# Transposes of the identity on TensorE between the second weight units and ahead of two later waits

## The reference

```python
# layer 1: attention of x [8, 8, 512, 64] with a state of 32 rows per head -> 4352 tokens of 512 values
# layer 2: soft mixture, 8 experts with 4 slots each (32 slots)
logits = x @ phi                        # [4352, 32]
d = softmax over the tokens (logits)
slot_input = (d.T @ x).reshape(8, 4, 512)
for e in range(8):
    h = np.maximum(slot_input[e] @ w1[e], 0.0)     # w1[e] 512 x 1024
    slot_out[e] = h @ w2[e]                        # w2[e] 1024 x 512
c = softmax over the slots (logits)
x = c @ slot_out
# layer 3: each token goes to the one expert that x @ w_gate names
out[mask] = gate_w * sigmoid(x @ w_output_gate)[e] * (np.maximum(x[mask] @ v1[e], 0.0) @ v2[e])
```

## Time and profile before

| | |
|---|---|
| median of three runs | 513.64 us |
| the profiled execution, whole | 512.83 us |
| its span, first to last instruction | 511.1 us |
| PE busy in the span | 452.8 us (89%) |
| mean clock granted to TensorE | 0.957 of full speed |
| data moved | 88.35 MB, mean 173 GB/s |

### The profile page before, as it was taken

How to read it: one execution, slowest core, us unless ns; L and a number is a source line. 1 busy time by engine, 2 the same in 40 slices (tenths; PEclk the granted TensorE clock), 3 DMA queues, 4 the chain that set the end, 5 groups by cost and what they waited for, 6 DMA issues and landing times.

```text
span 511.1 us, 10146 instructions
## 1 busy us (share of the span) xinstructions
PE 452.8 (89%) x3556; PEld 252.6 (49%) x3557; DVE 136.3 (27%) x278; ACT 143.9 (28%) x330; POOL 139.6 (27%) x207
## 2 busy tenths in 40 slices
PE   3788886799877949699999999999999999999991
PEld 3466664563415526544554545455454545545440
DVE  1489899830000894210101101010110101101000
ACT  3687764300000454321221212122121212212110
POOL 3153423046000122402323233232323323232110
PEclk9899999889797887999999999999999999999997
DMA  9879536748999979778674010110101011010110
GB/s 254 290 255 381 191 128 224 312 167 330 430 431 426 395 270 392 270 252 271 212 241 159 27 48 24 48 44 27 46 26 47 28 43 43 27 48 21 43 43 2
DMA packets 29378, 88.35 MB, mean 173 GB/s; under 512 B 6142, under 2 KB 15362, under 8 KB 26272
## 3 DMA queue, kind: packets, MB, share of 16 engines
q1 hardware_dynamic: 24304, 77.27, 40.8%
q0 software_dynamic: 3952, 10.33, 5.9%
q10 hardware_dynamic: 1088, 0.26, 0.3%
HBM read 77.61 MB, written 10.59 MB: 173 GB/s over the span
## 4 chain that ended last, share of the span: by engine, by line
PE 76%; DMA 8%; DVE 7%; issue 4%; ACT 2%; POOL 1%; SPq 0%; POOLq 0%; DVEq 0%; ACTq 0%
PE bank L874 48%; DMA arena<-in_moe_w 7%; PE bank L863 3%; PE bank L862 3%; PE bank L777 3%; PE bank L729 3%; PE bank L529 2%; PE bank L540 2%; PE bank L521 1%; DVE rsum L1120 1%; PE bank L557 1%; DVE rmx L1089 1%; DVE z L1093 1%; DVE nbias L1110 1%; PE bank L765 1%
## 5 line engine op out<-in xcount | busy, mean ns | idle before, releaser
L874 PE MATMUL bank<-arena,z 128*128 x560 | 249.2, 598 | 1.4 <-DVE z L1384 0.8
L874 PEld LDWEIGHTS bank<-arena,z 128*128 128x128 f32 x560 | 103.6, 190 | 122.5 <-issue 120.5
L1384 DVE TENSOR_SCALAR z<-bank 128x512 f32<-128x512 f32 x35 | 24.2, 691 | 251.3 <-PE bank L863 251.3
L1051 ACT ACTIVATE z<-bank,tile_gate 128x512 f32<-128x512 f32 x35 | 24.0, 687 | 228.3 <-PE bank L874 228.3
L460 POOL COPY rows_to<-sidx 128x1 int32 (+1 forms) x35 | 6.3, 181 | 152.9 <-ACT z L1051 152.9
L468 POOL DMA_INDIRECT z<-token_rows,rows_from x36 | 37.9, 1054 | 29.0 <-POOL rows_from L460 29.0
L478 POOL DMA_INDIRECT out<-z,rows_to x35 | 35.7, 1019 | 29.8 <-POOL rows_to L460 29.8
L862 PE MATMUL bank<-cT,parts 128*128 128x128 bf16 x280 | 36.4, 219 | 0.5 <-issue 0.5
L863 PE MATMUL bank<-cT,parts 128*128 128x128 bf16 x280 | 36.5, 219 | 0.0
L862 PEld LDWEIGHTS bank<-cT,parts 128*128 x280 | 27.4, 98 | 1.2 <-issue 0.9
L863 PEld LDWEIGHTS bank<-cT,parts 128*128 x280 | 27.4, 98 | 1.0 <-issue 0.5
(11 more groups left out here) (226 smaller groups left out, 498.4 us busy)
## 6 DMA issues: line engine op xcount, KB each, us to landing
arena<-in_moe_w SPq DMA_DIRECT2D x31, 2048.0 KB, 11.3
arena<-in_x SPq DMA_DIRECT2D x8, 1024.0 KB, 6.3
parts<-in_moe_w SPq DMA_DIRECT2D x1, 2048.0 KB, 8.6
token_rows<-z SPq DMA_DIRECT2D x8, 162.0 KB, 2.2
z<-token_rows,rows_from POOLq DMA_INDIRECT x36, 2.6
out<-z,rows_to POOLq DMA_INDIRECT x35, 2.9
z<-in_state ACTq DMA_DIRECT2D x4, 64.0 KB, 3.0
z<-in_state SPq DMA_DIRECT2D x4, 64.0 KB, 2.7
```

Of the source, the lines that this page charges most:

```text
L874: mm = e.matmul(pY[p][:, :], hT[p][:, c, :], arena[:, bass.ds(ex * UNIT + 512 * c, 512)], start=(c == 0), stop=(c == CF - 1))
L1051: e.activation(ysb[p], pY[p][:, :], ACT.Copy, scale=tile_gate[:, q:q + 1])\
L1384: e.tensor_scalar(hT[p][:, 4:8, :], bank[2 * p + 1][:, :].rearrange("p (c t) -> p c t", c=4), 0.0, None, ALU.max).then_inc(relu_v, 1)
```

## The change

Seven blocks of 14 transposes are put between the eight second units, 4 transposes behind the last of them (ahead of the wait for `so_copied`), and 4 ahead of the wait for `sot_ready`. Together 106 transposes are added. Nothing is removed and no wait is added.

```diff
                 mm.then_inc(w_used, 1)
+                if ex < NE - 1:
+                    keep_clock(14, pL)
+            keep_clock(4, pL)
             e.wait_ge(so_copied, 1)
             for c in range(CD):
                 mm = e.matmul(pT[:, P * c:P * c + P], every(soP, c, CD), fold[:, :, :], start=True, stop=True)
             mm.then_inc(sot_psum, 1)
 
+            keep_clock(4, pE)
             e.wait_ge(sot_ready, 1)
```

## The result

The changed kernel takes 518.31 us in the median of 11 runs (515.88 to 520.45), the kernel before 513.7 us in 11 runs beside it (512.11 to 515.71). The ratio is 1.0081, with a 95% interval of 1.0057 to 1.0106: the change costs 4.2 us (2.9 to 5.4). The forecast was 518.5.

What follows compares the result with a forecast made beforehand. The bound was the wait chain from second units through gate matmuls, DVE routing, table writes and unit 21's load to the tile loop. +7.3 - 0.5 - 1.4 - 0.4 = +5.0 us gave a forecast of 518.5, range 515.8 to 521.5.

Steps and rivals of the forecast that it cites:

- The step from unit 0 to unit 7: Second units on PE: the seven blocks of 14, less cover, start unit 7 at 161.7 against 154.36, 7.3 us later.
- The first block with its effect: Block behind unit 0: costs 2.5 us, ends at 140.7; unit 1 then runs at the high clock, giving back 0.7.
- The cover: PE's waits for the weights of units 6 and 7, 1.94 and 3.18 us, hide 5.1 us of the blocks.
- The two blocks of 4: Behind unit 7 and ahead of L759: they fit into 0.67 us waits and cost 0, at worst 0.2 each.
- The loads behind: DMA loads of units 16 to 20 don't suffer from the later second units; 10 us in hand.
- The clock's gain in L759 and L765: Gate matmuls on PE: clock high until some way into L765, gaining 0.5 us in L759 and 1.4 in L765.
- The path from L765 to the table writes: DVE's routing behind the gate matmuls: no gap, so L765's end moves the table writes by the same amount.
- Unit 21: PE after unit 21's load: the clock's rise may fall differently in the shifted stage; a gain of 0.4 us.
- The blocks cost half: Rival, blocks between second units: transposes at half of 0.11 us, 0.8 a block, kernel faster at 510.9; chance 0.06, later 0.05.
- Half hidden: Rival: later DMAs, or DVE and the table writes, absorb part; +1 to +3 us, 515 to 516.5; chance 0.07.
- The clock falls again before L765: Rival, gate matmuls: the thin matmuls lose the clock, +7.0 us, 520.6; chance 0.18.
- Transposes don't count for the clock: Rival, second units: all at the low clock, blocks 3.1 us and units 3.42, +28 us, 541; chance 0.03.

Runs made afterwards that it cites:

- e5: Changed kernel with 7 instead of 14 transposes in each of the seven blocks; 512.97 us, ratio 0.9978 to the kernel before.
- e8: Changed kernel with 28 instead of 14 transposes in each of the seven blocks; 528.59 us, ratio 1.0298 to the kernel before.
- e1: Changed kernel with only the two blocks of 14 ahead of real weight waits, and both blocks of 4; 510.66 us, ratio 0.9936 to the kernel before.
- e4: Changed kernel with blocks of 14 only behind the first five second units, and both blocks of 4; 514.55 us, ratio 1.0025 to the kernel before.
- e2: Changed kernel without blocks between the second units, only the two blocks of 4; 511.15 us, ratio 0.9981 to the kernel before.
- e3: Changed kernel without the two blocks of 4, only the seven blocks of 14; 520.47 us, ratio 1.0144 to the kernel before.
- e7: Changed kernel with only blocks of 14 and 24 between units, in the DMA waits, and 4, 4 and 6 behind; 509.75 us, ratio 0.9931 to before.
- e6: Changed kernel with each block of 14 transposes replaced by 7 identity matmuls of 16 columns; median 532.61 us, 518.04 to 538.33 in 8 runs.
- e9: Changed kernel without blocks between units, with 6 transposes added ahead of the g2_ready wait (4, 4 and 6); 511.55 us, ratio 0.9961 to before.
- e10: e7 timed again, beside e9; 509.88 us, ratio 0.9933 to the kernel before.

## Why the prediction was right

The price of the units and the cover for it held, and they make up most of the sum. Some smaller terms were wrong and cancelled; that part is luck.

- **The step from unit 0 to unit 7** was forecast at +7.3 us and measured +7.6. The first block with its effect put unit 1 at 5.97 us behind unit 0's start (143.24 - 137.27), against 5.9 in the account. A block with a unit takes 3.53 us, against 3.50, and that 0.03 six times over is most of the rest. The price came from nine other transposes among matmuls, and e5 and e8 confirm 0.11 us for each. Less the 2.47 us of this execution, unit 7 starts at 161.97, against 161.7.
- **The cover** was put at 5.1 us, all of it in two DMA waits. e1 shows that blocks inside them are free, e4 that early delay is absorbed in them.
- **The two blocks of 4** were counted at 0, and it is 0 (7.61 us ahead of L755 as at unit 7; e2).
- **The loads behind** didn't suffer, as forecast: the DMA share is 1.01 from 142.4 to 173.0. With double blocks (e8), which put unit 7 off by 18.6 us, the DMA engines do idle.
- **The clock's gain in L759 and L765**: 0.5 forecast and 0.58 measured (1.66 to 1.08), 1.4 forecast and 1.12 measured (4.24 to 3.12). The reason I gave was only half right. I named both the dense units and the filled waits; e3 has the dense units alone and gains nothing there, e2 has the filled waits alone and its trace has L767 at 2.70. The filled waits do it, but two of them don't promise it: e5 has both and its L769 took 4.24. So 1.12 is what this execution gave, between 0 and 1.91 in the traces of kernels with both blocks of 4.
- **The path from L765 to the table writes** was given as DVE's routing alone, with no gap. It also leads through the first `v1` units, where DVE waits 0.61 us for unit 16. I had them as slow as before and at no price. The wait stayed the same, so this costs nothing here; in e7 it is gone and part of the gain. The path was 0.34 us shorter in the changed kernel (8.07 to 7.73); its last DVE instruction took 0.22 us instead of 0.69, and why is open.
- **Unit 21** was forecast to gain 0.4 us. It gained more, 1.4 (from 6.64 us late at its start to 5.23 at the sort), since the clock rose 2.8 us after unit 21's start instead of 5.8. Ahead of that, the table writes and the landing took 1.07 us longer than before (5.57 late at the first write, 6.64 at the landing), which I had at 0. The two errors nearly cancel, and nothing in the prediction foresaw either. They are of the size by which executions of one kernel differ. From the sort on the loop gives back another 0.25 (5.23 to 4.98).
- **The rivals.** "The blocks cost half" is refuted by 0.11 us a piece. "Half hidden" had +1 to +3 us, of which the interval of 2.9 to 5.4 leaves only the edge, and unit 7 came the full 7.6 us later. "The clock falls again before L765" did not happen in the changed kernel's trace. It happened in e5's, and in e3, at 520.47, close to the 520.6 that it was priced at; e3 lacks the blocks of 4, though. "Transposes don't count for the clock" is refuted: in e8's trace 28 transposes of 3.27 us alternate with 1.7 us of unit, and the clock is 1.00 throughout. The rule in the Trainium skill ("TensorE: Matmul & The Clock Gate", Part 4: PE-mode transpose) doesn't hold for these float32 transposes. That its price of +28 us at the units is close to the 27 that e6 paid is because there, too, the units ran at the low clock throughout; e6 has no transposes among them.

## What to carry to other kernels

In this kernel filler work on PE was free only as long as the wait that it stood in; beyond that every transpose cost its full 0.11 us, since the list is executed in order whether there is a wait or not. So measure each wait in the trace, size the block to it, and put nothing where the engine runs back to back, even next to a wait that is real. Here the clock was kept for the thin matmuls by transposes in the waits right around them, in all three of these waits, and not by dense work long ahead. Look at the granted clock and not only at whether PE is busy: with 16-column matmuls as filler it was busy all the time and stayed at half clock (e6). And look at what else stands on the chain behind: here it was the first `v1` units.

## What the runs showed of the hardware

- PE busy for 52.47 of 52.50 us with 16-column matmuls between its units stayed at 0.50 of the clock (e6), and, going by the times and mean clocks, whether it did varied by execution: 8 runs of one program spread over 20 us.
- The weight load of a float32 128x128 block takes 333 ns at the low clock in the gate logits and 192 at the high one, but for the turn L752 it was 330 ns with the clock at 0.99 already, and L755 took 2.13 us at 1.00 as before. So the high clock brings this line nothing. The kernel reads these weights with a stride, and that may be the reason; no run changed it. The rows of the changed kernel (minimum, median, maximum ns):

```profile
L769 PEld LDWEIGHTS bank<-g2bd,parts x18: 186/192/333, 171.8 to 174.5; 128*128 128x128 f32 x16, 64*128 64x128 f32 x2
```

```profile
L755 PEld LDWEIGHTS bank<-fold,z x8: 308/329/329, 167.1 to 168.7; 128*128 128x128 f32 x8
```

- With transposes in all three waits behind the second units, the clock stayed at 1.00 for at least 22 us from unit 7 on in three traces (e7, e9, e10); with two of them filled it fell 7.1 to 10.0 us after unit 7's start, in six traces (the changed kernel, e1, e2, e4, e5, e8).
- Executions of one kernel differ by 4 us and more, in part along with the clock: of the changed kernel, those with a mean of 0.970 took 515.88 to 517.71 us and those with 0.961 took 518.99 and 520.45. But the profiled one had 0.967 and took 520.28.
